# Where the second layer's gate logits are computed in a three-layer kernel (local attention, two mixtures of experts)

## The reference, cut to what matters

```
x = attn(x, weight_gen)              # 7 taps per head, softmax over the taps; 2 x 3584 tokens, D = 192
# first layer, 8 experts, FF = 1024
logits = x @ w_gate; scale = log1p(exp(x @ w_noise)); noisy = logits + scale * noise
top2 of noisy, shares = softmax over the two
y = sum over the two of share[k] * (relu(x @ w1[e_k]) @ w2[e_k])
# second layer, 8 experts
logits2 = y @ w_gate2                # [N, 8]
e = argmax(logits2); out = softmax(logits2)[e] * (relu(y @ w1_2[e]) @ w2_2[e])
```

## Time and profile before

| | |
|---|---|
| device time, median of 3 runs | 1204.32 us (1201.09 to 1206.36) |
| profiled execution, its own time | 1202.42 us |
| its span, first to last instruction | 1200.1 us |
| mean granted clock of TensorE | 0.964 |
| busy: PE, PEld, DVE, ACT, POOL | 90%, 85%, 66%, 45%, 45% |
| bytes moved | 136.54 MB |

### The profile page before, as it was taken

How to read it: one execution, slowest core, us unless ns; L and a number is a source line. 1 busy time by engine, 2 the same in 40 slices (tenths; PEclk the granted TensorE clock), 3 DMA queues, 4 the chain that set the end, 5 groups by cost and what they waited for, 6 DMA issues and landing times.

```text
span 1200.1 us, 28811 instructions
## 1 busy us (share of the span) xinstructions
PE 1074.8 (90%) x7844; PEld 1024.5 (85%) x7845; DVE 789.8 (66%) x1381; ACT 542.1 (45%) x1072; POOL 536.1 (45%) x658
## 2 busy tenths in 40 slices
PE   3962999999999999999999999998999797999995
PEld 2541898989999999898999999998989697999995
DVE  9998889897677545555585545556556854656652
ACT  2340444454543444466344434456654443554542
POOL 1000466555444544434454545555444434655552
PEclk9985899999999999999999999999999998999998
DMA  7152223234223333538535333246766732543510
GB/s 247 54 165 73 69 90 115 91 101 130 79 87 86 96 91 113 164 96 205 127 89 101 93 90 108 77 125 196 205 155 110 154 104 83 150 123 102 145 41 22
DMA packets 105621, 136.54 MB, mean 114 GB/s; under 512 B 33834, under 2 KB 83821, under 8 KB 105324
## 3 DMA queue, kind: packets, MB, share of 16 engines
q1 hardware_dynamic: 86124, 92.99, 28.8%
q0 software_dynamic: 19456, 43.07, 12.7%
HBM read 104.78 MB, written 34.57 MB: 116 GB/s over the span
## 4 chain that ended last, share of the span: by engine, by line
PE 60%; DVE 15%; DMA 9%; issue 8%; ACT 3%; POOL 2%; DVEq 1%; ACTq 1%; POOLq 1%; PEldq 0%; SPq 0%
PE ps_y L1607 17%; PE ps_y L1608 8%; DMA row<-x_rows,read_now 7%; PE ps_h L1552 5%; PE ps_h L1556 5%; PE ps_h L1562 5%; PE ps_h L1559 5%; PE ps_h L1553 5%; DVE prod L640 4%; PE ps_x L1541 2%; PE ps_y L1619 2%; PE ps_x L1542 2%; DVE h_lo L972 2%; DVE prod L652 1%; DVE prod L857 1%
## 5 line engine op out<-in xcount | busy, mean ns | idle before, releaser
L1607 PE MATMUL ps_y<-w_hl,h_hi 128*128 128x384 f32 x1344 | 404.4, 366 | 7.4 <-DVE h_lo L972 6.8
L972 DVE SCALAR_TENSOR_TENSOR h_lo<-ps_h,h_hi 128x512 fp32r<-128x512 f32 x404 | 259.9, 686 | 189.1 <-ACT h_hi L1309 179.2
L1608 PE MATMUL ps_y<-w_hl,h_lo 128*128 128x192 f32 x1344 | 337.6, 251 | 0.0
L1309 ACT ACTIVATE h_hi<-ps_h 128x512 fp32r<-128x512 f32 x370 | 202.8, 596 | 226.7 <-PE ps_h L1562 218.8
L512 POOL DMA_INDIRECT row<-x_rows,read_now x202 | 227.7, 1127 | 121.2 <-POOL read_now L508 85.8
L1607 PEld LDWEIGHTS ps_y<-w_hl,h_hi 128*128 128x128 f32 x1344 | 253.7, 189 | 10.6 <-DVE h_lo L972 10.5
L1608 PEld LDWEIGHTS ps_y<-w_hl,h_lo 128*128 128x128 f32 x1344 | 257.6, 192 | 0.0
L1552 PE MATMUL ps_h<-xa_hi,w1a_hi 128*128 128x256 f32 x672 | 196.6, 292 | 3.9 <-issue 2.6
L1556 PE MATMUL ps_h<-xa_lo,w1a_hi 128*128 128x256 f32 x672 | 191.2, 285 | 0.8 <-DVE xa_lo L954 0.8
L1553 PE MATMUL ps_h<-xa_hi,w1a_lo 128*128 128x256 f32 x672 | 190.3, 283 | 1.3 <-issue 1.3
L1562 PE MATMUL ps_h<-xb_lo,w1b_hl 128*128 128x256 f32 x672 | 190.8, 284 | 0.0
(11 more groups left out here) (206 smaller groups left out, 1611.7 us busy)
## 6 DMA issues: line engine op xcount, KB each, us to landing
w_raw<-in_moe_w_dram SPq DMA_DIRECT2D x32, 768.0 KB, 5.0
w1a_raw<-in_moe_w_dram SPq DMA_DIRECT2D x32, 512.0 KB, 3.5
w1b_raw<-in_moe_w_dram SPq DMA_DIRECT2D x64, 256.0 KB
x_rows<-tok SPq DMA_DIRECT2D x21, 384.0 KB, 7.1
x_pad<-in_x_dram SPq DMA_DIRECT2D x2, 2688.0 KB, 10.2
x_pad<-y_rows SPq DMA_DIRECT2D x14, 384.0 KB, 4.0
prod<-y_rows SPq DMA_DIRECT2D x14, 384.0 KB, 5.4
row<-x_rows,read_now POOLq DMA_INDIRECT x202
```

What stands on the lines that cost most here:

```text
L972: nc.vector.scalar_tensor_tensor(out=h_lo[:, i * GF:(i + 1) * GF, :], in0=ps_h[:, i, :].rearrange("p (f t) -> p f t", f=GF), scalar=0.0, i ...
L1309: act.activation(h_hi[:, i * GF:(i + 1) * GF, :], ps_h[:, i, :].rearrange("p (f t) -> p f t", f=GF), ACT.Relu).then_inc(h_hi_ready, 1)
L1607: nc.tensor.matmul(ps_y[:, u, 0:2 * D], h_hi[:, i, cols], w2_hl[b][:, f, :], start=(i == 0), stop=False)
L1608: last = nc.tensor.matmul(ps_y[:, u, 0:D], h_lo[:, i, cols], w2_hl[b][:, f, 0:D], start=False, stop=(i == FC - 1))
```

## The change

The logits of the second layer are (sum of share times y_k) times G. Since y_k = h w2, y_k G = h (w2 G), so eight more columns, w2 G, are put beside w2 of the first layer.

- `w2_hl` becomes 2 x 200 wide instead of 2 x 192 (`DE` = D + E). In passes 0 and 1 a `down` pair has 400 and 200 columns instead of 384 and 192; `y`, `y_lo`, and the rows of `y_rows` have 200 elements, and the loads, weighting and scatter with them. Passes 2 and 3 keep 384 and 192, read with a stride.
- w2 G of the eight experts is made in the starting part. SP loads each first-layer w2 a second time (`stage_w2`: 1024 runs of 512 bytes and 1024 of 256 bytes an expert), experts 0 and 1 early, 2 to 5 into `x_pad` after `x_used`, 6 and 7 behind that. PE turns each (`turn_w2`: 12 transposes of 128 x 128), ACT copies the three PSUM banks back (three copies of 512 columns), PE multiplies (`gates_of_w2`: 4 + 8 fp32 products of 16 and 8 columns). On PE this stands between the logits and `find_rows`, with `counts(0)` behind the third expert's. ACT does it behind `logarithm(0)`; `soft(1)` moves behind it.
- SP loads chunk 1 of x, and all that follows in its queue, after the last expert's w2 is turned. POOL clears a part of `x_pad` again.
- ACT (`place_gates`) and DVE (`split_gates`) put 64 columns into `w2_hl` with each expert of passes 0 and 1.
- In passes 1 and 2 `stage_columns`, `turn_columns`, `read_turned`, `score_columns` and `score` go. `combine_logits` (two DVE operations over 224 elements) adds up the two experts' weighted logits. `SCORE`, `COUNT`, `MARK` and `LIST` of these passes are one tile earlier.
- In the diff the first `turn_w2` is ACT's and the second PE's; `TURNED_EARLY` is 3.
- `tap_stat` and the second `h_rows` buffer move into other buffers.

```diff
+    DE = D + E
-        SCORE = tuple(LAST[p] + 2 for p in range(PASSES - 1))
+        SCORE = (LAST[0] + 2, LAST[1] + 1, LAST[2] + 1)
...
             def load_chunk(c):
                 if c > 0:
-                    sp.wait_ge(x_used, c)
+                    sp.wait_ge(w2_turned_ps, E)
...
+            for e in STAGED_FIRST:
+                stage_w2(e)
+            for g in range(NB):
                 store_block(0, g)
+                if g == NB - 2:
+                    sp.wait_ge(x_used, 1)
+                    for e in STAGED_NEXT:
+                        stage_w2(e)
+            for e in range(len(STAGED_FIRST) + len(STAGED_NEXT), E):
+                sp.wait_ge(w2_turned_ps, e - 5)
+                stage_w2(e)
             load_chunk(1)
...
+            def combine_logits(p):
+                step = stepper(dve, f"logit_step{p}")
+                c = p - C
+                step(nc.vector.tensor_tensor(a_lane[:, :, :], results[1][:, :, D:DE],
+                                             share[c][:, 1, :].unsqueeze(2).broadcast_to(wide), ALU.mult))
+                step(nc.vector.tensor_tensor(value[:, :, :], results[0][:, :, D:DE], a_lane[:, :, :], ALU.add))
...
+            def turn_w2(e):
+                act.wait_ge(w2_turned_ps, e + 1)
+                if e == 1:
+                    act.wait_ge(x_used, 1)
+                if e > 1:
+                    act.wait_ge(gates_ps, e - 1)
+                for to, part in zip(w2_turned[e % 2], ps_turned[e % 2]):
+                    last = act.activation(to, part, ACT.Copy)
+                last.then_inc(w2_turned_in, 1)
...
             logarithm(0)
+            for e in range(TURNED_EARLY):
+                turn_w2(e)
+            read_counts(0)
+            for e in range(TURNED_EARLY, E):
+                turn_w2(e)
+            read_gates()
             soft(1)
-            read_counts(0)
...
+            def turn_w2(e):
+                pe.wait_ge(w2_staged_in[e], 32)
+                if e > 1:
+                    pe.wait_ge(w2_turned_in, e - 1)
+                raw, (a0, a1, b) = w2_staged[e], ps_turned[e % 2]
+                for f in range(FC):
+                    nc.tensor.transpose((a0, a1)[f // 4][:, f % 4 * P:(f % 4 + 1) * P], raw[:, f * P:(f + 1) * P], ident[:, :])
+                for i in range(FC // 2):
+                    last = nc.tensor.transpose(b[:, i * P:(i + 1) * P], raw[:, FC * P + i * P:FC * P + (i + 1) * P], ident[:, :])
+                last.then_inc(w2_turned_ps, 1)
+            def gates_of_w2(e):
+                pe.wait_ge(w2_turned_in, e + 1)
+                a0, a1, b = w2_turned[e % 2]
+                for i in range(FC // 2):
+                    nc.tensor.matmul(ps_gates[:, e, 2 * i:2 * i + 2, :], b[:, i * P:(i + 1) * P], gate_w_b[1][:, :, :], start=True, stop=False)
+                    for f in (2 * i, 2 * i + 1):
+                        last = nc.tensor.matmul(ps_gates[:, e, f, :], (a0, a1)[f // 4][:, f % 4 * P:(f % 4 + 1) * P], gate_w[1][:, :],
+                                                start=False, stop=(f % 2 == 1))
+                last.then_inc(gates_ps, 1)
...
             front(0, range(NB + 1))
-            counts(0)
+            for e in range(E):
+                turn_w2(e)
+                if e == TURNED_EARLY:
+                    gates_of_w2(e - 1)
+                    counts(0)
+                elif e > 0:
+                    gates_of_w2(e - 1)
+            gates_of_w2(E - 1)
             find_rows()
             transpose_rows(0)
+            pe.wait_ge(gates_low, 1)
```

212 lines of the change are left out of this document (128 added, 84 removed).

## The result

The changed kernel takes 1240.21 us (median of 4 runs, 1235.79 to 1243.45) beside 1202.70 us of the kernel before on the same chip: a ratio of 1.030, 95% interval 1.027 to 1.033. The prediction was 1194 us, range 1182 to 1216; it had the wrong sign. The profiled execution took 1239.0 us (span 1237.2), 36.6 us more than the one before (1202.42).

What follows compares the result with a forecast made beforehand. The prediction took PE, with 60% of the chain, to bound the kernel: 1202.4 - 25 (scoring removed, steps earlier) + 7 (wider columns) + 9.5 (starting part) = 1193.9, given as 1194 us, range 1182 to 1216.

Steps and rivals of the forecast that it cites:

- What bounds the kernel: Whole kernel: PE holds 60% of the chain, so in the passes each us taken from PE is a us saved.
- Starting part, +9.5 predicted: Starting part: new turning and gates of w2 G make it 9.5 us longer, 5 if DVE and PE overlap better.
- That is the very mix that the change adds, and it speaks for a clock that rises by some 90 us and holds: Starting part: transposes and scoring passes ran at clock 1.00 from 543.30 to 546.40 us, so the new work should too.
- Rival 1: Starting part: clock stays at 0.50 through the new phase, lists end 37.6 us later, 1222 us; chance 0.2.
- the saving of 25: Passes 1 and 2: removed scoring and earlier steps save 12 + 10 + 3 = 25 us, bounds 15 and 37.
- Columns, +7.0: Passes 0 and 1: wider down pairs, 400 columns for 384, cost 7.0 us over 952 pairs; 10.5 if all count, 0 if hidden.
- Pass 1, a gain of 12: Pass 1, eight tiles with side work: removing turning and scoring saves 12 us, bounds 9 and 15.
- no tile of pass 1 waits for rows: Pass 1: the argument against the saving of passes 1 and 2 being lost to gathers.
- Rival 2: Passes 1 and 2: saving lost to gathers in both, 15 us instead of 25, 1204 us, no change; chance 0.12.
- Pass 2, a gain of 10: Pass 2, eight tiles: 10 of 18.7 us saved, the rest becoming waits for rows; bounds 6 and 16.
- One tile earlier, a gain of 3: Steps after scoring, mainly pass 2's half tile: marks leave j = 14, saving 3 us, bounds 0 and 6.
- Staged w2 late, rival 4: Starting part: staged w2 arrives late because its runs are short, lists near 143 us, 1214 us; chance 0.05.

Runs made afterwards that it cites:

- e8: Changed kernel with each gate product 64 identity columns wide, w2 G not made, only the starting part read; pass 0 starts at 136.25 us.
- e13: Changed kernel with gate weights padded by zeros to 64 columns a product, right w2 G, padding built behind the attention's products; 1213.28 us, ratio 1.007.
- the repetition: The changed kernel run again unedited; 1235.28 us, ratio 1.024 to the kernel before.
- e18: Changed kernel with 64-column gates, earlier counts and lists, earlier chunk 1, later expert 1 weights, two columns a tile in pass 1, old pass 2 SCORE; 1195.18 us, 0.992.
- e1: Changed kernel without making w2 G, chunk 1 loaded as before; pass 0 starts at 124.33 us; 1174.94 us, not comparable because of other routing.
- e11: Changed kernel loading only the first expert's y rows in pass 2, half the y bytes; pass 2 takes 211.2 us instead of 214.3.
- e16: Changed kernel with each second-layer weight load moving an eighth of its bytes; pass 2 takes 191.6 us instead of 214.3.
- e15: Changed kernel with the steps behind scoring in pass 2 at their old tile numbers; 1223.13 us, ratio 1.015.
- e4: Changed kernel with counts(0) directly behind the first gates and find_rows batches between the turns of experts 3 to 6; 1233.75 us, ratio 1.024.
- e12: Changed kernel with each expert's transposes done three times and one 64-column product for its twelve gate products, only the starting part read; pass 0 at 140.28 us.
- e5: Kernel of e4 with the load of chunk 1 waiting for the turn of expert 5 instead of expert 7; 1229.75 us, ratio 1.020.

## Why the prediction was wrong, step by step

- **What bounds the kernel**: right for the plain tiles. "A us taken from PE is a us of the time as long as nothing else comes last" was the condition that failed in passes 1 and 2.
- **Starting part, +9.5 predicted, +27.2 measured: the largest error.** The failed step is "That is the very mix that the change adds, and it speaks for a clock that rises by some 90 us and holds". It did rise, at 87.8 us, and fell again at 91.2; from 83.6 to 137 us its mean was 0.60. The earlier trace rows show 3 us of the mix at 1.00 between full-width products; they show holding for that long and no more. I had looked at the busy share of PE, which is near 1.00 in both, and not at what streams through it. e8 and e13 show the price: with the clock held, pass 0 starts at 134.7 to 136.3 us, so 14 to 15 of the 27 us are the clock (20 to 21 in the repetition). At the lists, which DVE takes at 121.28 us in e13 and at 140.13 in the changed kernel, it is 18.9; the first rows of e13 give 3.7 of it back. Rival 1 had the mechanism with a chance of 0.2, and the time was above its 1222 although its +37.6 was too much, since the saving of 25 was gone as well.
- **The rest of the starting part**: with the clock held e13 starts pass 0 11.9 us behind the kernel before, where I had 9.5, and by its steps: gates 7 end at 117.3 (forecast 117.4), the lists are taken from PE at 121.28 instead of 113.18, 8.1 later (forecast 8.7). Only the first rows are 3.8 us later still, where I had put 0.8 for their meeting "the last of the weights". That is what they meet: chunk 1 has landed at 124.8, the gather goes out at 124.74 and is used at 132.61, 7.9 us later, and the weights of expert 1 are on their way beside it; in e18, which holds them back, it is 4.2 us. The working for a clock of 1.00 was right; the clock was not.
- **Columns, +7.0**: the plain tiles are 9.93 and 7.90 us, where I had 9.92 and 7.78 for 400 columns that count and 200 that are hidden, and 9.98 for all of them. 55 x 0.13 + 9 x 0.18 = 8.8 us, inside the bounds; right but for the half tiles.
- **Pass 0** took 3 us more than its columns explain (28 x 0.13 + 4 x 0.18 = 4.4 of 7.2). The first tile is 1.2 us longer, at the low clock for 6.1 us of it and not 3.6. Tiles 3 and 4, at the change to the second pair of experts, take 13.91 and 12.43 us (11.23 and 12.32 before; 11.57 and 12.60 in e1). PE stands idle for 2.18 us ahead of tile 4, and no row names a releaser for it; open.
- **Pass 1, a gain of 12**: with 4.4 for the columns the profile shows 3.7 (328.3 to 329.0), the repetition 7.5, the other runs with four columns 4.5 to 12, so the size of the loss is partly chance. "no tile of pass 1 waits for rows" was true of the kernel before and said nothing on tiles that are 1.9 us shorter. I had seen the gather's pace in pass 2 and not worked out the same for pass 1, where the y loads are the same. Rival 2 named it, with 0.12, and for half of the saving.
- **Pass 2, a gain of 10**: 3.6 us in the eight tiles, where my own argument (11.5 to 12.5 us for a gather beside the loads) stood; it should have gone to the end of its range, 6 or less. What I blamed, y loads and stores, gave 3 us at most for half of the loads (e11); nearly all of the weights gave 23 (e16), and I had left them out.
- **One tile earlier, a gain of 3**: the sign was wrong, +4 (e15). The half tile's wait did shrink, from 5.61 to 3.68 us as forecast to "some 3", but it is 3.97 in e15 too, without the earlier steps, so that proves nothing for them. Places and marks now stand with an expert's weight splits in tiles 76 and 77, which take 32.0 us instead of 22.9. The 4.41 us of waiting for rows in tile 77 come with them; that the store of the scales, issued at 968.66 just ahead of that gather and of weight loads, has a part in it is argued and wasn't tried.
- **Staged w2 late, rival 4**: PE never stands idle ahead of a turn of w2 in any run.
- **The two costs together** are what no single rival held: rival 1 and rival 2 at once. I had given them as alternatives, 1222 and 1204; added on top of each other (the start at +27.2, the columns at +8.8, no saving) they give 1238.

## What to carry to other kernels

Before work is taken off an engine that is busy all the time, compare the bytes that a tile must move with the time that the tile will then have; an engine's side work may be what spaces the transfers. Products with few columns on fully loaded weights were not cheap here, since the clock fell during them: widening them to 64 columns with zeros cost no time and kept it up. Other widths weren't tried. And when something is made earlier, look at what it will now meet, in the queues and in the DMA engines; the earlier lists of e4 won nothing until the load of chunk 1 was moved too.

## What the runs showed of the hardware

- A busy share near 100% in the profile goes with either granted clock. In the changed kernel's new phase, with 24 passes of 8 or 16 columns and 12 transposes an expert, PE is 100% busy at 0.50 to 0.67; with 64 columns the clock is 1.00. At the full clock the products start 0.112 us apart at either width.
- fp32 transposes of 128x128 with next to nothing between them hold the full clock (1.00 from 90 to 117 us in e12, having risen from 0.50 at 88.4).
- The same program differs by its clock from execution to execution: in the starting part 0.67 or 0.50 in the stretch from 100 to 110 us, and pass 0 at 149.96 or 156.13.
- An indirect gather of 256 rows, from POOL's first issue to PE's turning them, took 4.2 us with no large load in flight (118.88 to 123.06, e18), 6.3 (e5) and 7.9 us (e13) beside the last of 1.8 MB of weights, and 11.5 us beside a load of 2.7 MB that had just begun (e4).
